# A fused attention, SoLU and gated-product kernel: a seventh part buffer with new turns, one more low half on GpSimd, and the last pair's tokens requested in two halves

## What is computed

```python
def _moe2_ref(x, w_in, w_out):          # x: 3072 x 512, w_in: 512 x 2048, w_out: 2048 x 512
    h = x @ w_in
    relu6 = np.clip(h + 3.0, 0.0, 6.0)
    g = h * relu6 / 6.0
    return (g @ w_out).astype(np.float32)
```

## Time and profile before

| | us |
|---|---|
| median of 3 runs | 943.51 |
| lowest, highest | 942.12, 944.47 |
| the profiled execution, its own time | 945.21 |
| its span | 943.4 |
| TensorE matmul busy in the span | 907.4 (96%) |
| VectorE busy | 684.1 (73%) |
| ScalarE busy | 471.7 (50%) |
| GpSimd busy | 267.2 (28%) |
| granted TensorE clock, mean | 0.985 of full |

### The profile page before, as it was taken

The page is one execution under the profiler, slowest core; times in us unless marked ns, Lnnn a source line. Parts: engine busy times, 40 slices in busy tenths (PEclk is TensorE's granted clock), DMA queues, the critical chain, the costliest instruction groups (busy, mean ns, idle before and its releaser), DMA issues.

```text
span 943.4 us, 17258 instructions
## 1 busy us (share of the span) xinstructions
PE 907.4 (96%) x6200; PEld 811.4 (86%) x6200; DVE 684.1 (73%) x1095; ACT 471.7 (50%) x1092; POOL 267.2 (28%) x317
## 2 busy tenths in 40 slices
PE   8887999999999999999999999999899999999998
PEld 7666888989888888888978888888689999999997
DVE  3898688878777777857585555555688978878783
ACT  4555465555556565625575555455544333333320
POOL 5452165554422353551103332233420000000000
PEclk8988999999999999999999999999999999999999
DMA  8723336566754376468453233333967434344441
GB/s 191 157 56 62 93 77 174 155 178 178 217 129 133 109 195 163 151 210 331 148 216 139 104 133 133 133 133 114 359 257 282 140 105 157 108 139 130 136 138 45
DMA packets 146907, 146.46 MB, mean 155 GB/s; under 512 B 96936, under 2 KB 107176, under 8 KB 145832
## 3 DMA queue, kind: packets, MB, share of 16 engines
q1 hardware_dynamic: 134328, 100.55, 36.8%
q0 software_dynamic: 7920, 38.94, 11.6%
q10 hardware_dynamic: 4608, 6.29, 1.9%
HBM read 90.05 MB, written 55.71 MB: 154 GB/s over the span
## 4 chain that ended last, share of the span: by engine, by line
PE 75%; DVE 13%; DMA 6%; ACT 3%; issue 2%; POOL 1%; SPq 1%; ACTq 0%; DVEq 0%; POOLq 0%
PE banks L858 22%; PE banks L1042 21%; PE banks L901 20%; PE banks L812 3%; DMA g_scratch<-part 3%; PE banks L781 2%; DVE prob L1301 2%; PE banks L838 2%; PE banks L825 2%; DVE gs L1277 2%; PE banks L849 2%; DVE gs_raw L1457 1%; DMA k_in<-in_k_dram 1%; DMA x_mix_scratch<-x_mix 1%; DMA xs_raw<-x_mix_scratch 1%
## 5 line engine op out<-in xcount | busy, mean ns | idle before, releaser
L1042 PE MATMUL banks<-vs,gs 128*128 128x256 f32 x2016 | 243.3, 283 | 2.5 <-DVE o_stage L1491 1.5
L1042 PEld LDWEIGHTS banks<-vs,gs 128*128 128x128 f32 x2016 | 242.3, 192 | 3.5 <-DVE o_stage L1491 1.7
L901 PE MATMUL banks<-xs,ws 128*128 128x512 f32 x1008 | 233.2, 392 | 6.1 <-ACT part L1139 4.3
L901 PEld LDWEIGHTS banks<-xs,ws 128*128 128x128 f32 x1008 | 189.2, 189 | 48.6 <-issue 4.6
L1237 ACT CAST gs<-gs_raw 128x1792 fp32r<-128x1792 f32 x48 | 81.4, 1695 | 132.2 <-DVE gs_raw L1457 132.2
L858 PE MATMUL banks<-y_t,w_out 128*128 128x384 f32 x768 | 140.9, 338 | 1.3 <-DVE y_t L1277 1.3
L858 PE MATMUL banks<-w_in,x_t 128*128 128x512 f32 x552 | 133.8, 398 | 1.1 <-DVE solu L1331 1.1
L858 PEld LDWEIGHTS banks<-y_t,w_out 128*128 128x128 f32 x768 | 132.1, 188 | 2.2 <-issue 1.7
L858 PEld LDWEIGHTS banks<-w_in,x_t 128*128 128x128 f32 x552 | 103.6, 191 | 23.3 <-DVE solu L1331 1.4
L1090 ACT ACTIVATE prob<-score,small 96x128 f32<-96x128 f32 x256 | 99.2, 392 | 19.2 <-DVE small L1290 19.2
L1457 DVE TENSOR_TENSOR gs_raw<-gs_raw 128x256 f32<-128x256 f32 x192 | 81.4, 424 | 30.4 <-DMA gs_raw<-g_scratch 25.5
(11 more groups left out here) (88 smaller groups left out, 1064.9 us busy)
## 6 DMA issues: line engine op xcount, KB each, us to landing
g_scratch<-part SPq DMA_DIRECT2D x96, 256.0 KB, 2.1
gs_raw<-g_scratch SPq DMA_DIRECT2D x45, 512.0 KB, 3.9
q_in<-in_q_dram SPq DMA_DIRECT2D x32, 192.0 KB, 4.0
x_scratch<-x_out ACTq DMA_DIRECT2D x32, 192.0 KB, 1.9
out_dram<-o_stage SPq DMA_DIRECT2D x12, 512.0 KB, 5.7
k_in<-in_k_dram SPq DMA_DIRECT2D x24, 240.0 KB
v_in<-in_v_dram SPq DMA_DIRECT2D x24, 240.0 KB
v_split_scratch<-v_split POOLq DMA_DIRECT2D x3, 1792.0 KB, 7.8
```

The lines of the kernel that those rows point to most:

```text
L901: mm = pe.matmul(ps, ws[:, W_OF[i], a, kc, :], xs[g][X_OF[i]][:, m, kc, :], start=(fresh and x == 0), stop=(x == len(passes) - 1), skip_gr ...
L1042: mm = pe.matmul(m_ps[i][:, s, :], gs[x][:, a, G_OF[i], s * P:(s + 1) * P], vs[p][:, m, V_OF[i], :], start=(p == 0 and s == 0 and y == 0), ...
```

## The change

1. **Seven part buffers.** C11 (s1) and C22 (s3) share buffers 0 to 2, C12 (s2) turns through 3 to 5, C21 always takes the new buffer 6. `stores_of` tells how many stores each buffer has seen after so many units, for the waits that need all of them.
2. **Group 0's tokens, the seam before the product stage.** Operand 5 is split after the stage's high and low halves of `y_t`, no more ahead of them.
3. **Group 2's tokens.** GpSimd requests 0 and 6 at once as before, but 2 only after product 7 and 1 only after product 4 of unit (0,1). The order of splitting becomes 0, 4, 5, 6, 1, 3, 2, and each split and mix moves to another place: operand 0 is split one place earlier, ahead of the mixes of 5, 6 and 3.
4. **`VFIRST` 3 for 2.** GpSimd makes the low half of `vs[2]` too; VectorE's `low_vs(2)` goes.

```diff
-    VFIRST = 2
+    VFIRST = 3
+    NPART = 7
-        part = [at(f"part{e}", 172 + 2 * e, [P, XT], F32) for e in range(6)]
+        part = [at(f"part{e}", 172 + 2 * e if e < 6 else 205.75, [P, XT], F32) for e in range(NPART)]
-        stored = [sem(f"stored{e}") for e in range(6)]
+        stored = [sem(f"stored{e}") for e in range(NPART)]
-        X_ORDER = [(0, 1, 5, 6, 4, 3, 2), (0, 1, 2, 6, 5, 4, 3), (0, 5, 1, 6, 4, 3, 2)]
+        X_ORDER = [(0, 1, 5, 6, 4, 3, 2), (0, 1, 2, 6, 5, 4, 3), (0, 4, 5, 6, 1, 3, 2)]
         def part_of(p, g, what):
-            k = 4 * g + PART[what] - (0 if type(p) is int and p == 0 else 4)
-            return k % 6, 2 * p + k // 6
+            x = g if type(p) is int and p == 0 else (g - 1) % 3
+            q = 0 if type(p) is int and p == 0 else p + (g - 1) // 3
+            if what == "s1":
+                return x, 2 * q + x // 2
+            if what == "s3":
+                return (x - 1) % 3, 2 * q + (1 if x else 0)
+            return (3 + x, q) if what == "s2" else (6, nth(p, g))
+
+        def stores_of(e, units):
+            if e == 6:
+                return units
+            first, second = (units + 2 - e % 3) // 3, (units + 1 - e % 3) // 3 if e < 2 else (units + 2) // 3
+            return first + second if e < 3 else first
...
-            for i in (0, 6, 2, 1):
+            for i, done in ((0, None), (6, None), (2, 7), (1, 4)):
+                if done:
+                    pool.wait_ge(prod_done[done], nth(0, 1) + 1)
                 pool.dma_start(xs_raw[2][i][:, :, :], x2_block(2, i)).then_inc(x_here[2][i], 16)
...
                     if last and kk == 3:
-                        for n in range(3):
+                        for n in range(2):
                             high_xs(0, n)
...
                     if last and kk == 4:
-                        high_xs(0, 3)
+                        for n in (2, 3):
+                            high_xs(0, n)
                         keep(0, 0, "s1", 1)
...
-            unit(0, 1)
-            unit(1, 0, then={1: lambda: high_xs(2, 0), 6: lambda: high_xs(2, 1), 7: lambda: high_xs(2, 2)})
-            unit(1, 1, then={1: lambda: high_xs(2, 3), 6: lambda: high_xs(2, 4), 7: lambda: high_xs(2, 5)})
-            unit(1, 2, then={1: lambda: high_xs(2, 6)}, refill=True)
+            unit(0, 1, then={7: lambda: high_xs(2, 0)})
+            unit(1, 0, then={1: lambda: high_xs(2, 1), 6: lambda: high_xs(2, 2), 7: lambda: high_xs(2, 3)})
+            unit(1, 1, then={1: lambda: high_xs(2, 4), 6: lambda: high_xs(2, 5), 7: lambda: high_xs(2, 6)})
+            unit(1, 2, refill=True)
...
             unit(0, 1, then={22: lambda: mix_xs(0)})
-            unit(1, 0, then={0: lambda: mix_xs(1), 12: lambda: mix_xs(2), 11: lambda: mix_xs(3),
-                             22: lambda: low_xs(2, 0)})
+            unit(1, 0, then={0: lambda: low_xs(2, 0), 12: lambda: mix_xs(1), 11: lambda: mix_xs(2),
+                             22: lambda: mix_xs(3)})
...
             sum_of(PAIRS, 0, 12)
-            low_vs(2)
             gate(PAIRS, 0, 12)
```

More of the change, by code:

```diff
@@ L139, in attention_solu_hardswish @@
         held = [at(f"held{x}", 198 + 2 * x, [P, 2, GH], F32) for x in range(2)]
-        assert base + int(205.75 * KB) <= nc.sbuf_usable_end
+        assert base + int(207.75 * KB) <= nc.sbuf_usable_end
         smax = small[0:TQ, 0:8]
@@ L271, in attention_solu_hardswish @@
         W_OF = {1: 0, 2: 1, 7: 2, 4: 3, 5: 4, 6: 5, 3: 6}
-        PART = {"s1": 0, "s2": 1, "s3": 2, 21: 3}
         XM_OF = {6: 0, 4: 1, 5: 2, 3: 3}
-        X_ORDER = [(0, 1, 5, 6, 4, 3, 2), (0, 1, 2, 6, 5, 4, 3), (0, 5, 1, 6, 4, 3, 2)]
+        X_ORDER = [(0, 1, 5, 6, 4, 3, 2), (0, 1, 2, 6, 5, 4, 3), (0, 4, 5, 6, 1, 3, 2)]
         W_ORDER = (1, 6, 2, 7, 5, 4, 3)
@@ L488, in _ @@
             sp.wait_ge(prod_done[3], 3 * PAIRS)
-            for e in range(6):
-                sp.wait_ge(stored[e], 16 * 14)
+            for e in range(NPART):
+                sp.wait_ge(stored[e], 16 * stores_of(e, nth(last, 1)))
             load_gs(3)
@@ L511, in _ @@
                 if n == 6:
-                    for e in range(6):
-                        sp.wait_ge(stored[e], 16 * 2 * PAIRS)
+                    for e in range(NPART):
+                        sp.wait_ge(stored[e], 16 * stores_of(e, 3 * PAIRS))
                     load_vs(7)
@@ L762, in _ @@
             pool.wait_ge(prod_done[3], nth(PAIRS - 1, 0) + 1)
-            for e in range(6):
-                pool.wait_ge(stored[e], 16 * 12)
+            for e in range(NPART):
+                pool.wait_ge(stored[e], 16 * stores_of(e, nth(PAIRS - 1, 0) - 2))
             load_step(0)
@@ L1135, in keep @@
                     act.wait_ge(stored[e], 16 * used)
-                elif e >= 4:
+                elif e in (4, 5):
                     act.wait_ge(x2_free[e - 4], 16 * (1 + 2 * NG))
@@ L1392, in batch @@
                     if last and kk == 3:
-                        for n in range(3):
+                        for n in range(2):
                             low_xs(0, n)
                     if last and kk == 4:
-                        low_xs(0, 3)
+                        for n in (2, 3):
+                            low_xs(0, n)
                         sum_of(0, 0, 11)
```

## The result

| | before | after |
|---|---|---|
| median, us | 944.47 of 7 runs (942.12 to 946.30) | 940.11 of 7 runs (938.23 to 941.46) |
| the profiled execution, us | 945.21 | 938.23 |
| its span, us | 943.4 | 936.4 |
| granted TensorE clock, mean | 0.985 | 0.985 |

The ratio after to before is 0.9954, with a 95% interval of 0.9937 to 0.9971: 4.3 us faster (2.7 to 5.9). The profiled execution is the fastest of its seven, so the two profiles lie 7.0 us apart.

The account below looks back on a forecast made before the run. TensorE was taken as full in the product stage's body (157.00 of 157.00 us), leaving gains only at three seams: 1.28 + 0.5 + 2.5 = 4.3 us off a 943.5 us median gives 939.2, range 937.0 to 942.3.

Parts of the forecast that it names:

- The body gains nothing and gets no wait: Product stage, 501 to 658: TensorE busy 157.00 of 157.00 us, so new buffer turns can gain nothing there.
- First seam: TensorE's wait before 440.54 for the low half of `y_t` goes whole: gain 1.28 us, bounds 0 and 1.28.
- Second seam: Waits before 477.43 and 479.29: two tokens requested later gain 0.5 of 1.43 us, bounds 0 and 1.43.
- Third seam, item 1: C21 of (7,1): gate 1.32 us earlier, half a microsecond of wait left before product 7, no clock fall behind it.
- Item 2: After product 4 of (7,2): weights 1 and 6 land 1.3 us sooner; TensorE idles 1.9 us for weight 1.
- Item 3: C21 of (7,2) waits for nothing; product 7 of (8,0) starts at 683.55, not 687.40: 3.85 us.
- Item 4: Clock likelier falls after the 1.9 us idle before weight 1: 1.7 lost, 0.7 hidden, minus 1.0 us.
- Item 5: `vs[2]` on GpSimd: worth nothing, but slows a VectorE gate before the last C21 store; minus 0.3 us, bounds 0 and 0.6.
- the clock stays up: Rival: no clock fall at the wait before weight 1, so 1.0 us comes back: 938.2 us; chance 0.2.
- The weights land when they did: Rival: earlier issue of weights 1 and 6 buys nothing beside GpSimd's V loads; sum 2.9 us, 940.6; chance 0.18.
- The change only moves the third seam's wait: Rival: weight 7, 5 or 4 of (8,0) is late next; sum 1.8 us, 941.7; chance 0.12.
- Tokens 2 and 1: Rival: these tokens come too late for unit (1,0), 4.6 us lost plus 1.7 for the clock: 945.5; chance 0.08.

Follow-up runs that it names:

- The control: The changed kernel run again without an edit; 938.2 us median of 8, ratio 0.9936 to the kernel before.
- Experiment 6: The changed kernel with all four token loads of pair 1 requested at once again, new split order kept; 938.62 us, ratio 0.9939.
- the V2 kernel: The kernel before with only V2's low half moved to GpSimd, six part buffers; 944.06 us, ratio 1.0013.
- experiment 7: The changed kernel with V3's load requested later by GpSimd, between its pieces of V0 and V1; 946.3 us, ratio 1.0015.
- the seven-buffer kernel: The kernel before with only the seven part buffers, their turns and their waits; 938.2 us median of 10, ratio 0.9962.
- 8: The changed kernel with V3's load requested later by GpSimd and V2's low half back on VectorE; 941.94 us, ratio 0.9978.
- 12: The changed kernel with V3's load later from SyncE and a 64 KB transfer issued by GpSimd between its pieces; 946.69 us, ratio 1.0045.
- experiment 9: The changed kernel with V3's load requested from SyncE behind the last weight of split 8; 936.58 us median of 6, ratio 0.9936.
- 10: The changed kernel with V3's load later from SyncE and g step 1's low half behind the sum of C12 (7,2); 936.08 us, ratio 0.9909.

## Why the prediction came out right

The time was forecast at 939.2 and measured at 940.11; the sum of 4.3 us equals the gain by the ratio. That is partly luck. The control found 6.0 us (3.7 to 8.4), and the stretches from the first product on say more than 4.3 as well. Step by step:

- **The body gains nothing and gets no wait.** Right: 154.00 of 154.00 us busy.
- **First seam, 1.28.** Right against before's profile: its wait of 1.28 went, and the stretch fell by 1.51. As the price of the part it is one draw: in the five profiles with the old order the wait was 0 to 1.91 us, once with a fall of the clock behind it, and the stretch 0.1 to 3.7 us longer than in the new order. Operand 5 moved without a cost that these profiles show.
- **Second seam, 0.5 of 1.43.** Right in place and a little low: 16.43 to 15.33 in the first pair, 0.7 as a mean of the groups (six profiles at 16.07, eight at 15.34). Experiment 6 shows that the later requests do it. The 0.5 was reasoned from VectorE's wait for token 6, which went from 1.59 to 0.71 here but is as short in other profiles with the old requests; what went every time is TensorE's wait for weight 2.
- **Third seam, item 1.** Right: C21's gate no longer waits, product 7 of (7,2) waits 0.44 us (half a microsecond was forecast), and the clock stays up. The body shortened by 1.5 us; the term was 1.32.
- **Item 2, "I take 1.3 off both landings".** This is the term that was mis-sized. On the prediction's scale (from the start of the body, 479.29 before and 477.29 now) weight 1 was issued 1.65 us sooner, near the 1.3, but landed 6.7 sooner; weight 6 was issued 0.70 sooner and landed 5.8 sooner. Counted from the start of product 7 of (7,2), weight 1 landed at 6.55 before (9.7 us after its issue at 668.98) and at 1.45 now (4.6 after 665.33), weight 6 at 9.91 and 5.79. I had moved the issue and kept the time on the way. But V1 goes out only 0.25 us sooner on that scale, so weight 1 is now issued 0.35 us ahead of V1, where it was 1.05 behind it, and its store is 0.72 ahead where it was 0.67 behind. In all nine profiles with seven buffers weight 1 stands ahead of V1 and takes 4.2 to 5.3 us; in all five with six it stands behind and takes 9.3 to 10.5. The order of issue was not varied by itself. The forecast wait of 1.9 us for weight 1 never came; a wait of 1.77 for weight 2 did, and no term of the sum had it.
- **Item 3, nothing waits at C21 of (7,2).** Right: the 2.26 us before product 7 of (8,0) are gone.
- **Item 4, a fall of the clock, minus 1.0.** Wrong. All four profiles with seven buffers and V3 early have one wait of 1.77 to 2.56 us there, and the third seam is 15.4 us plus that wait: nothing is lost to the clock. All five with six buffers have at least one fall, behind the wait of 1.7 to 1.9 us or behind the one before product 7 of (8,0): their seams are 1.75 to 3.6 us longer than 15.4 plus their waits. Windows of 4 us, from before, the V2 kernel and experiment 7 (after 9.03 us of waiting, 5 us):

```profile
672.00:676.00 4.00, 3.83 (x10) 3.02 (x11) 4.00 (x4) 3.22 (x5) 2.22 (x2) 0.57 1.00 405
```

```profile
686.00:690.00 4.00, 4.00 (x13) 3.14 (x12) 1.65 (x2) 1.44 (x4) 4.00 (x6) 0.57 0.35 131
```

```profile
693.00:698.00 5.00, 5.00 (x14) 3.97 (x15) 2.64 (x6) 1.41 (x2) 0.00 (x0) 0.57 0.29 108
```

  A wait of 1.88 before product 7 of (7,2) left the clock up in the V2 kernel (its 18 matmuls took 4.39 us) and one of 1.83 took it down in before's (5.96). So the length of the wait does not decide it here, and what does stays open.
- **Item 5, V2 on GpSimd, minus 0.3.** Worth nothing before the last stage: right. A cost in the time is not told from nothing. The slower gates are there as forecast: the last two that ScalarE's relu releases before the mixes take 1.29 and 1.12 us in the changed kernel and 0.72 and 0.69 in the seven-buffer kernel. And there is one effect that was not forecast: beside GpSimd's pieces the four mixes of a g step take 3.06 us, and 1.79 without.

```profile
686.30 3.06 DVE L1474 TENSOR_TENSOR gs_raw<-gs_raw 128x256 f32<-128x256 f32 x4
```

```profile
685.48 1.79 DVE L1468 TENSOR_TENSOR gs_raw<-gs_raw 128x256 f32<-128x256 f32 x4
```

  The Trainium skill's rule (SBUF — State Buffer, "Who interferes with whom") is that the two exclude each other for a whole instruction, from which the prediction took that a gate waits one piece at most. In the changed kernel the trace agrees (gates of 1.1 to 1.3 us); in experiments 7, 8 and 12 it does not: 10.61, 5.87 and 10.62 us are 14, 7 and 14 pieces.

Together, where the sum had 2.5 us for the third seam, the first pair of profiles shows 1.64 (body) + 3.61 (third seam) - 0.25 (last stage) = 5.0, and the means of the four six-buffer and the four seven-buffer profiles of the table 1.5 + 4.2 - 0.5 = 5.2. The last stage's share is that it now starts before its first steps are ready: 0.20 us before its 85th matmul in the changed kernel is a wait for a low half of `gs` that before did not have. With 1.5 and 0.7 for the other seams the mean profile has gained 7.4 us, more than the 4.3 and 6.0 by the ratios. Both intervals (to 5.9 and to 8.4) and the start-up's scatter leave room for most of that, not surely for all of it; with one profile for each kernel it stays open.

Rivals: "the clock stays up" is what happened, at the third seam. "The weights land when they did" is refuted by 4.6 against 9.7 us; its text has the V loads "ahead of weight 1 in both orders", and they are not. That also speaks against the use I made of the Trainium skill's rule (DMA: Bandwidth & Descriptors, "Queues, rings and completion order") that a DMA engine takes its queues in turn, packet by packet. No run here tests the rule itself, but an issue that passes from behind two of three large loads to ahead of all three went with a landing 5 us sooner. "The change only moves the third seam's wait" has a grain of truth, weight 2's 1.77 us in the place of 5.1 us. Tokens 2 and 1 held nothing up: in the changed kernel no engine waits for them in unit (1,0). A slip in the range: its lower end, 937.0, is put down to a case whose own sum is 937.3.

## What to carry to other kernels

When a step frees an engine's queue, ask which transfers change places in the queues, not only how much sooner they are issued: a weight that went out just ahead of three 0.9 MB loads landed in 4.6 us, and one behind the first two of them in 9.7. Before adding a buffer, look for a large load in the busy stretch that nobody wants yet; moving one, later and to another engine's queue, gave about half of what the whole change gave. And judge an effect of a few us by stretches between fixed events, over several profiles, since a start-up that nobody touched moved by 6.7 us here.

## What the runs showed of the hardware

- **A VectorE operation can be held up by a whole run of GpSimd operations.** A gate with two operands in SBUF that began 0.14 to 0.15 us after GpSimd had begun to issue a transfer (0.57 us), with more GpSimd pieces of 0.69 us right behind, ended 0.55 to 0.56 us after the last of them: 10.61, 5.87 and 10.62 us for 14, 7 and 14 pieces, three times out of three. GpSimd's pieces ran at full pace meanwhile (0.69 us each; 20.51 us for 21 in experiment 9, where the two engines took turns). No profile without such an issue between the pieces has a gate over 1.29 us. The Trainium skill (SBUF — State Buffer, "Who interferes with whom") calls the port pair that the two engines share an exclusive lock: whoever issues first gets it for the whole instruction, and the other blocks. A wait over many instructions goes beyond that. Whether the transfer's issue must coincide with the gate's start was not varied.
- **The granted clock** fell after waits of 1.8 us in some profiles (0.57 behind 1.83 us) and held after waits of 1.88 (same place of the program) and up to 2.56 us (ten us later) in others (1.00).
- **Landing times scatter** by 2 to 2.5 us for the same request, issued at the same place behind the same loads (V1: 6.7 and 9.1 us; V2: 9.3 and 11.3, experiments 9 and 10, which differ only in a later step of VectorE).
